# Moving a 32x32-block transpose of attention probabilities off the matmul engine, with the loops unrolled

## The reference

```
scores = q @ k.T / 8
thresh = max(scores) - tau
e      = exp(where(scores >= thresh, scores, -1e9) - max(scores))
x      = (e / (sum(e) + 1e-9)) @ v            # [2304, 512] after joining the heads
h = x @ w_in                                  # 512 -> 2048
x = (max(h,0) + alpha * min(h,0)) @ w_out     # 2048 -> 512
out = (((x @ w1) * (x @ w2)) @ w3) @ w_out2   # 512 -> 1024 -> 1024 -> 512
```

## Time and profile before

| | us |
|---|---|
| runs of the kernel (3) | 1110.12, 1111.26, 1111.39; median 1111.26 |
| profiled execution: span | 1110.1 |
| work around that span, taken as the rest to the fastest run | under 0.1 |
| steps (first maximum to the first matmul behind the steps) | 14.55 to 534.12 |
| stages behind the steps | 534.12 to 1110.1 |

### The profile page before, as it was taken

The page is one execution under the profiler, slowest core; times in us unless marked ns, Lnnn a source line. Parts: engine busy times, 40 slices in busy tenths (PEclk is TensorE's granted clock), DMA queues, the critical chain, the costliest instruction groups (busy, mean ns, idle before and its releaser), DMA issues.

```text
span 1110.1 us, 21790 instructions
## 1 busy us (share of the span) xinstructions
PE 1050.7 (95%) x7504; PEld 946.4 (85%) x7504; DVE 515.7 (46%) x1341; ACT 459.9 (41%) x1130; POOL 496.5 (45%) x665
## 2 busy tenths in 40 slices
PE   3899978999997999999899999999999999999998
PEld 2677755778786877878889999999999999999998
DVE  4777677768675676763444333334311111111111
ACT  4777677767764666753222222222221112111111
POOL 4866678857664575733333444444321112112111
PEclk9999999999998999999999999999999999999999
DMA  6454456342424224211533333336320111111000
GB/s 172 111 151 146 136 142 193 103 114 59 127 81 121 76 74 130 76 50 49 195 110 133 136 126 125 125 125 276 138 97 22 64 43 35 50 64 43 21 21 21
DMA packets 42912, 113.21 MB, mean 102 GB/s; under 512 B 7632, under 2 KB 18896, under 8 KB 38608
## 3 DMA queue, kind: packets, MB, share of 16 engines
q1 hardware_dynamic: 35472, 98.59, 27.4%
q10 hardware_dynamic: 7360, 13.63, 4.1%
HBM read 79.70 MB, written 32.51 MB: 101 GB/s over the span
## 4 chain that ended last, share of the span: by engine, by line
PE 81%; DVE 7%; ACT 4%; issue 3%; DMA 2%; POOL 2%; SPq 0%; ACTq 0%; POOLq 0%; DVEq 0%
PE psum L702 21%; PE psum L739 18%; PE psum L633 11%; PE psum L688 10%; PE psum L579 6%; PE psum L564 5%; PE psum L546 5%; PE psum L646 4%; DVE mx L922 2%; DVE e_ring L941 2%; DVE g_raw L962 1%; ACT e_ring L801 1%; DMA raw_e<-weights 1%; ACT pt_rest L821 1%; DVE g_raw L968 1%
## 5 line engine op out<-in xcount | busy, mean ns | idle before, releaser
L1064 POOL TENSOR_TENSOR g<-g_raw,g 128x288 fp32r<-128x288 f32 x192 | 154.3, 804 | 355.7 <-ACT g L905 234.2
L739 PE MATMUL psum<-xy,w_a 128*128 128x288 f32 x1536 | 204.5, 295 | 0.7 <-DVE y_buf L1045 0.7
L739 PEld LDWEIGHTS psum<-xy,w_a 128*128 128x128 f32 x1536 | 203.5, 188 | 1.0 <-issue 1.0
L1102 POOL TENSOR_SCALAR p_ring<-e_ring,rden,uni 128x512 f32<-128x512 f32 x144 | 114.2, 793 | 115.3 <-DVE rden L947 103.5
L546 PE MATMUL psum<-ks,qs 128*128 128x288 f32 x640 | 127.9, 328 | 24.4 <-POOL qs L1064 13.2
L941 DVE SCALAR_TENSOR_TENSOR e_ring<-psum,thr,e_ring 128x576 f32<-128x576 f32 x144 | 117.3, 815 | 60.6 <-ACT e_ring L801 53.8
L922 DVE TENSOR_REDUCE mx<-psum 128x1 f32<-128x576 f32 x144 | 108.7, 755 | 70.3 <-PE psum L546 70.1
L902 ACT COPY g_raw<-psum 128x288 f32<-128x288 f32 x64 | 25.5, 399 | 235.2 <-PE psum L739 235.2
L546 PEld LDWEIGHTS psum<-ks,qs 128*128 128x128 f32 x640 | 96.4, 202 | 26.7 <-issue 20.4
L564 PE MATMUL psum<-ident,p_ring 128*128 128x128 f32 x576 | 92.4, 285 | 21.7 <-ACT pt L821 11.9
L801 ACT ACTIVATE e_ring<-psum,nb 128x576 f32<-128x576 f32 x144 | 106.8, 742 | 14.6 <-POOL p_rest L1106 9.9
(11 more groups left out here) (74 smaller groups left out, 1391.0 us busy)
## 6 DMA issues: line engine op xcount, KB each, us to landing
xy<-xs SPq DMA_DIRECT2D x16, 1152.0 KB, 5.5
k_raw<-k SPq DMA_DIRECT2D x32, 288.0 KB, 4.4
q_raw<-q SPq DMA_DIRECT2D x32, 288.0 KB, 5.6
xs<-x_hl SPq DMA_DIRECT2D x64, 144.0 KB, 1.8
ys<-xy SPq DMA_DIRECT2D x8, 1152.0 KB, 4.2
xy<-ys SPq DMA_DIRECT2D x8, 1152.0 KB, 5.1
raw_w<-weights SPq DMA_DIRECT2D x34, 256.0 KB, 2.8
raw_w<-weights ACTq DMA_DIRECT2D x18, 256.0 KB, 3.0
```

The source lines that it names most:

```text
L739: last = mm(psum[:, 2 * ab + f % 2, 0:CH], w_a[:, wp, slot, (f % 4) * P:(f % 4 + 1) * P], xy[c][:, xp, kt, :], start=(n == 0), stop=(n == ...
L1064: sub = lambda out_, a, hi: nc.gpsimd.tensor_tensor(out_, a, hi.bitcast(F32), ALU.subtract)
L1102: nc.gpsimd.tensor_scalar(p_ring[:, t % 4, :], e[:, 0:MAIN * P], r, n_, ALU.mult, ALU.add)
```

## The change

1. No identity matmuls, no copies of them by ACT. DVE transposes every 32x32 block of a tile (`transpose_of`, three steps behind the scores) from `e_ring` (now six deep, scaled in place by one POOL instruction of 576 columns) into `ybuf`. When the nine tiles of a pair are there, SP moves the blocks to their partitions with 16 DMAs from SBUF to SBUF (`move_blocks`, position 2), each from 32 partitions to 32 partitions, with rows of 288 float32 (1152 bytes), four or five to a partition: 2304 rows, 2.65 MB for a pair. `zbuf` is single; the move of a pair waits for the previous product with v.
2. The product with v stands at positions 7, 8 and 0 (steps 25, 26, 27 of pair 0; two, two and one key blocks), five steps behind the move. The order of the tiles in a pair puts the mixed one in the middle. `SHARE` is `[0, 3, 2, 3, 3, 2, 3, 0, 0]` by position.
3. The activation: ACT computes relu(-h), DVE adds (1 - alpha) times that to h: one instruction each instead of two on DVE.
4. The small operations move: threshold to ACT, fallback and epsilon to POOL (128x1 each).
5. The DMAs of early weight pieces and of the product move from ACT's queue to SP's.
6. DVE masks the previous tile behind the new tile's maximum, not before it.
7. All loops are unrolled. Two waits (`s_ye`, `s_oe`) are added ahead of `down`.

```diff
-SHARE = [2, 0, 2, 2, 2, 2, 2, 2, 2]
+SHARE = [0, 3, 2, 3, 3, 2, 3, 0, 0]
+E_RING = 6
+LEAD = 9
+LAG_T = 3
+LAG_PV = 25
+LAG_X = LAG_PV + 3
...
+            def move_blocks(n):
+                sp.wait_ge(s_t, TILES * (n + 1))
+                if n >= 1:
+                    sp.wait_ge(s_pv, 2 * n)
+                cols = slice(y_start(n), y_start(n) + WIDE)
+                for c in range(QD):
+                    tiles = len(range(c, KB, QD))
+                    for a in range(QD):
+                        sp.dma_start(zbuf[c * SQ:(c + 1) * SQ, 0:tiles, a, :],
+                                     ybuf[a * SQ:(a + 1) * SQ, c:KB:QD, cols]).then_inc(s_z, 16)
...
+                if kt == 0:
+                    pe.wait_ge(s_v_in[par], 32 * (n // 2 + 1))
+                    pe.wait_ge(s_z, 16 * QD * QD * (n + 1))
...
+            def transpose_of(t):
+                n, i = divmod(t, TILES)
+                dve.wait_ge(s_norm, t + 1)
...
+                nc.vector.transpose(ybuf[:, :, at:at + SQ],
+                                    e_ring[:, t % E_RING, :].rearrange("p (b c) -> p b c", c=SQ)).then_inc(s_t, 1)
...
+            def negative_of(cc, f, h):
+                act.wait_ge(s_h, FT * cc + (f + 1))
+                if f >= 2:
+                    act.wait_ge(s_gl, FT * cc + (f - 1))
+                nc.scalar.activation(g_raw[:, f % 2, :], h, ACT.Relu, scale=-1.0).then_inc(s_neg, 1)
...
+            def activation_of(cc, f, half, h):
+
+                a = FT * half + f
+                dve.wait_ge(s_neg, FT * cc + (f + 1))
+                nc.vector.scalar_tensor_tensor(g_raw[:, f % 2, :], g_raw[:, f % 2, :], beta_sb[:, a:a + 1], h,
+                                               ALU.mult, ALU.add).then_inc(s_g, 1)
...
+            def probs_of(t):
+                i = t % TILES
+                pool.wait_ge(s_rden, t + 1)
+                pool.wait_ge(s_uni, t + 1)
+                e = e_ring[:, t % E_RING, :]
+                nc.gpsimd.tensor_scalar(e, e, rden[:, i:i + 1], uni[:, i:i + 1], ALU.mult, ALU.add)\
+                    .then_inc(s_norm, 1)
```

More of the change, by code:

```diff
@@ L39 @@
 TILES = 2 * MAIN + 1
-TB = PAIRS * TILES
-GROUPS = 2 * MAIN + 3
+NT = NPAIR * TILES
 HALF = SEQ // 2
@@ L224, in build @@
         block = ctx.enter_context(nc.Block())
[L227 to L238, removed]
-            with engine.Fori(2, BATCH) as b:
-                step(b)
-            step(BATCH)
-        def steps_of(b):
-            return TB if not isinstance(b, int) or b < BATCH else SPAN + START + 3
@@ L504, in _ @@
-            with sp.Fori(0, NCH // 2 - 1) as b:
-                second_half(b)
-            second_half(NCH // 2 - 1, last=True)
-            def stage_2(b, last=False):
-                for c in range(2):
-                    ck = 2 * b + c
-                    if not last:
-                        sp.wait_ge(s_ab, 2 * FT * (ck + 1))
-                        load_chunk(ys, ck + 2, c)
-                    sp.wait_ge(s_oe, KD * (ck + 1))
-                    sp.dma_start(out[ck], y_buf[:, :, :]).then_inc(s_out, 16)
@@ L517, in _ @@
-            with sp.Fori(0, NCH // 2 - 1) as b:
-                stage_2(b)
-            stage_2(NCH // 2 - 1, last=True)
+            for ck in range(NCH):
+                c, last = ck % 2, ck >= NCH - 2
+                sp.dma_start(y_buf[:, :, :], yp[ck]).then_inc(s_yp_in, 16)
+                if ck < NCH - 1:
+                    load_pieces((EARLY + N_M1) // 2 + 1 + ck)
+                if ck == NCH - 2:
+                    for m in range(2):
+                        sp.wait_ge(s_wc_out[m], 16 * FT // 2)
+                    sp.dma_start(w_c[:, :, :, :].bitcast(F32), wc).then_inc(s_wc_in, 16)
+                sp.wait_ge(s_yl, KD * (ck + 1))
+                sp.dma_start(ys[ck], xy[c][:, :, :, :].bitcast(F32)).then_inc(s_ys, 16)
+                sp.wait_ge(s_ys, 16 * (ck + 1))
+                load_chunk(ys if last else xs, c if last else ck + 2, c)
@@ L520, in _ @@
+            for ck in range(NCH):
+                if ck + 2 < NCH:
+                    sp.wait_ge(s_ab, 2 * FT * (ck + 1))
+                    load_chunk(ys, ck + 2, ck % 2)
+                sp.wait_ge(s_oe, KD * (ck + 1))
+                sp.dma_start(out[ck], y_buf[:, :, :]).then_inc(s_out, 16)
             sp.wait_ge(s_out, 16 * NCH + 16)
@@ L823, in x_hi @@
-            def x_hi(b, u, part):
-                act.wait_ge(s_pv, count(b, u, 2, part + 1))
-                if part == 0 and (not isinstance(b, int) or b * PAIRS + u >= 1):
-                    act.wait_ge(s_xs, count(b, u, 64, 0))
+                if t == 0:
+                    act.wait_ge(s_tau, 1)
+                nc.scalar.activation(thr[:, i:i + 1], mx[:, i:i + 1], ACT.Identity, bias=ntau[:, 0:1])\
+                    .then_inc(s_thr, 1)
+            def x_hi(n, part):
+                act.wait_ge(s_pv, 2 * n + part + 1)
+                if part == 0 and n >= 1:
+                    act.wait_ge(s_xs, 64 * n)
```

939 lines of the change are left out of this document (409 added, 530 removed).

## The result

| | before | after |
|---|---|---|
| runs, median (us) | 1110.97 (4 runs) | 1220.5 (1219.21 to 1221.98, 4 runs) |
| ratio, 95% interval | | 1.0981, 1.0963 to 1.0999 |
| profiled span | 1110.1 | 1217.8 |

The account below looks back on a forecast made before the run. PE was taken to bound the kernel, busy 95%. Early pairs +10, pairs 6 to 15 -21, tail -1 and the rest 0 took 1110 to 1098 profiled, 1099 us forecast; forecast's own range 1086 to 1108, wider range 1050 to 1142.

Parts of the forecast that it names:

- PE's part: Inside the steps: 26.3 us of PE work a pair without identity matmuls, 25.7 built up from single rows.
- rival D: PE's clock falls at the product with v, or straight code comes late: 1115 to 1150 us; chance 0.07.
- Rival C: DVE's transpose takes 1.4 us, about 3.4 us for each of 15 pairs: 1149 us; chance 0.08.
- POOL's part: Inside the steps: scaling 0.85 us, two 128x1 operations 0.35 each, 1.55 a step; POOL latest in "h" pairs.
- POOL gives back 1 by lagging: In "h" pairs of pairs 6 to 15, POOL's lagging takes 1 us off 30.7, leaving 29.7 us.
- The moves: 16 DMAs a pair land in 13.4 us; PE waits 1.0 ("y"), 0 ("h"), 1.7 us (early pairs).
- Rival B: Moves land late and PE waits at position 7; at 16 us the time is 1129 us; chance 0.20.
- Early, +10: Pairs 1 to 5: 147 us, plus waits for moves (6) and weight pieces (5): 158 against 147.8.
- Pairs 6 to 15, -21: "h" pairs at 29.7 us and "y" pairs at 28.1 sum to 286.3 against 307.0, unrolling included.
- Tail, -1: End of the steps: units 26.2, product with v 5.8, last move's wait 4, some 0.5: 36.5 against 37.7 us.
- ACT hidden everywhere, so 0: Whole kernel: ACT loses the copies and gains little work, all hidden behind other engines, so 0 us.
- behind the steps, 0: Stages behind the steps stay at 576 us, "h" matmuls covering ACT's activation; without cover, two chunks lose about 1 us each.

Follow-up runs that it names:

- The second experiment: Early weight pieces and product stores issued by ACT, not SP: 1220.0 us in the changed kernel, 1184.8 us with the y stores on ACT too.

## Why the prediction was wrong, point by point

The step that failed is the list of what the change makes wait. The sum has two waits in the steps, PE's for the moves and ACT's for weight pieces in pairs 1 to 5, and none behind them. It left out the y stores in SP's queue (measured: 33 us) and the loop through the two buffers of `g_raw` (28 us), and it had the moves too quick for the step at which PE wants them (a step later gave 32).

- **PE's part.** PE's work is about right: pair 14 has 25.6 us busy, where 26.3 and 25.7 were computed. But a smaller load on PE was worth nothing while others held it. The sum also took PE at full clock throughout (see rival D).
- **DVE's part.** Right. The transpose has a mean of 760 ns, 144 times, where 0.76 was taken. Rival C is out.

```profile
L834 DVE STREAM_TRANSPOSE ybuf<-e_ring 128x576 f32<-128x576 f32 x144 | 109.5, 760 | 4.7 <-POOL e_ring L961 4.7
```

- **POOL's part.** Prices right: 834 ns for the scaling (0.85 taken), 330 and 229 for the small ones (0.35 taken for each). "POOL gives back 1 by lagging" in "h" pairs failed: it can't lag, because ACT's relu waits for POOL's subtraction of two tiles before. Forecast 29.7, measured 33.4; with four buffers 29.2 to 29.9.
- **The moves.** 13.4 us from trigger to use were taken; 15.65 was measured in pair 13, 15.65 to 16.2 in the "y" pairs, and 19.1 in pair 1 of the kernel with the pieces on ACT. An issue took 0.69 us or more, not 0.57. The sum let the bytes of all moves set the time. The short moves show that the issues set most of it: 12.0 us with a ninth of the bytes. By the lower of the two rates that the Trainium skill has for 32 partitions (SBUF — State Buffer, "Door 1: The DMA port swizzle"), 189 GB/s, the sum would have had 15.6 us. The number agrees with the 15.65 measured; that this rate is what set it, no run shows. The higher of the two rates of the Trainium skill, 218 GB/s, is a little under the 225 that the earlier trace rows show for loads to 64 partitions, so these rows bear it out only roughly. Rival B had a late landing as its cause and, at 16 us, this landing. It asked 30 us in all for it; a step later gave 31.8 (with new shares), fewer bytes 41.6. So the size of B was about right and its chance, 0.20, too low; that the two numbers are so near is in part luck, since B knew nothing of the issues.
- **Early, +10.** +30.4. The sum took the pieces' wait (5) and the moves' (6) as separate. The second experiment shows that they are not: take the pieces out of SP's queue and the moves land later. Short moves gave 25 us in pairs 1 to 6.
- **Pairs 6 to 15, -21.** +59.0, so 80 us more than forecast. The five "y" pairs' wait behind the y stores is 33.6 of them: the sum named the pieces of weights but not the y stores, two to six positions later in the same queue, nor that a copy waits for them ahead of ACT's exponential. Pair 6 is 17.4 of them: 29.7 was forecast, with no piece in it, and ACT waits 12.66 us for one. The other four "h" pairs are 15.3 (POOL's part, above). Another 13.4 are left in the "y" pairs without the wait for the y stores; with the product a step later the "y" pairs took 21 less.
- **Tail, -1.** +6.6. PE waited 6.4 us for the last move, where 4 was taken, and was busy 37.9 us at a granted clock of 0.88, where 32.5 was summed up.
- **"ACT hidden everywhere, so 0"** and **behind the steps, 0.** +9.5 behind the steps, and the "h" pairs at 33.4 us. I gave it "two chunks, about 1 us each if the cover went". The cover was 1.62 us a tile; the loop through ACT, DVE and POOL needs 1.72, in all ten chunks with this activation. It cost 14 us there; that only 9.5 show is because the rest of the change, unrolling among it, makes these stages 4.8 us shorter (571.2 with DVE's activation against 576.0). A sum over each engine's busy time can't show that: none but PE is busy over 30%.
- **Unrolling, 6.3 us at the jump in the steps.** Right, rather low: 1102.0 against 1112.2 for all loops; pair 10 alone gave 7.6. It is a gain that needs none of the rest of the change.
- **Rival D.** Partly there. Slow stretches go with PE's pauses (0.87 in pair 13, 0.65 in pair 5 above), and the same 178 matmuls of a "y" pair take 28.1 us busy there against 24.6 at 1.00 in the kernel with short moves. The mean clock of the runs rises as the waits are mended (0.94 to 0.97), so it goes with them; what it costs beside them was not separated by a run. That straight code comes late, the other half of this rival, is out: unrolling alone made the kernel before 9 us faster.

Taken one by one, the mends are worth 33 us (y stores), 3 (pieces), 28 (four buffers) and 32 (a step later). DVE's activation behind gave 13.5 by itself, but 6 on top of four buffers (577.2 to 571.4 behind the steps). That makes some 102 of the 109.5 between the two medians; all together gave 107.0. The exchange, against the unrolled kernel before, is then slower by 11 to 12; in that are also the small operations moved and ACT's activation within the steps, which were not taken back.

## What to carry to other kernels

When a change puts a block of issues into a DMA queue, list everything behind it in that queue, with the position at which it is due, and for each the engine that waits for it and what stands behind that wait. Check a chain over several engines as a loop: the sum of its instructions round the buffer's reuse, divided by the tiles in flight, against the time the bound engine takes for a tile; busy shares don't show it. A gain in matmul time that is paid in DMAs has to be priced by their number as well as by their bytes: one queue issues them one behind the other, and everything behind them waits for all. And each bundled part (unrolling, here) should be timed by itself.

## What the runs showed of the hardware

- Moves from 32 to 32 partitions within SBUF (1152-byte rows, 180 or 144 KB each) landed 4.1 to 4.8 us after issue by the median, and 16 of them took 15.65 to 16.2 us from the first issue to their use in the "y" pairs of the change. With rows of 128 bytes they landed after 1.9 us, and 16 took 12.0 to 12.8. So 2.65 MB in 15.65 us is what this train of DMAs delivered; that it is a limit of the DMA engines, no run shows.
- 16 such issues took 11.0 to 12.0 us in the change (0.69 to 0.75 each), 10.3 to 11.5 with the short rows, and 13.9 (0.87 each) in an early pair with weights loading from ACT's queue.
- A DVE transpose of 32x32 float32 blocks over 576 columns costs 760 ns, what a subtraction of that size costs (754 ns).
- Opening a loop that ran 6% over PE's pace gained 9 us in the stages behind the steps, and the same edit 4 us in each "h" pair, where POOL's scaling and split stand in the loop too.
